# Delta-rule recurrence and two expert layers on one core: joins of the triangular solve in half as many products, the router's weights stored by rows, a longer run of filler products in the routing, and the state's turn ahead of the corner product

## The reference

```python
for t in range(S):
    y[:, :, t] = einsum('bhd,bhde->bhe', r, state)
    Sa = einsum('bhde,bhe->bhd', state, a)
    state = state * w[:, :, None, :] - einsum('bhd,bhe->bhde', Sa, b) + einsum('bhd,bhe->bhde', v, k)
...
e_idx = argmax(x @ w_gate, axis=1)
out[mask] = gate_w[mask, None] * eom[mask, e, None] * (maximum(x[mask] @ w1[e], 0.0) @ w2[e])
...
x = _moe_ref(x=x, **moe_kwargs)
return _moe2_ref(x=x, **moe2_kwargs)
```

## Time and profile before

| | us |
|---|---|
| median of 3 runs | 1289.96 |
| lowest, highest | 1289.43, 1297.5 |
| the profiled execution | 1287.04 |
| its span | 1285.3 |
| PE busy | 1097.9 (85%) |
| VectorE busy | 558.7 (43%) |
| ScalarE busy | 396.4 (31%) |
| GpSimd busy | 302.4 (24%) |

### The profile page before, as it was taken

The page is one execution under the profiler, slowest core; times in us unless marked ns, Lnnn a source line. Parts: engine busy times, 40 slices in busy tenths (PEclk is TensorE's granted clock), DMA queues, the critical chain, the costliest instruction groups (busy, mean ns, idle before and its releaser), DMA issues.

```text
span 1285.3 us, 41335 instructions
## 1 busy us (share of the span) xinstructions
PE 1097.9 (85%) x18328; PEld 949.7 (74%) x18328; DVE 558.7 (43%) x864; ACT 396.4 (31%) x550; POOL 302.4 (24%) x253
## 2 busy tenths in 40 slices
PE   1189894888898889986899999999569999997997
PEld 0188784777888878885788888888448888876885
DVE  6635363364536443416176777767650111110111
ACT  0033332333333334331333333333004333323330
POOL 5440443043034213000112122121201212121111
PEclk8557997896888689777799999999868999998999
DMA  3333439343334333216024224333300331443000
GB/s 84 93 96 84 101 88 68 78 95 81 95 74 110 81 88 74 56 40 199 18 74 146 66 77 129 98 115 103 87 7 29 123 107 61 141 139 112 21 11 1
DMA packets 143115, 107.64 MB, mean 84 GB/s; under 512 B 91553, under 2 KB 120233, under 8 KB 142813
## 3 DMA queue, kind: packets, MB, share of 16 engines
q1 hardware_dynamic: 130560, 84.99, 25.0%
q0 software_dynamic: 6016, 16.05, 3.9%
q10 hardware_dynamic: 6364, 3.96, 2.0%
HBM read 87.51 MB, written 22.09 MB: 85 GB/s over the span
## 4 chain that ended last, share of the span: by engine, by line
PE 76%; DVE 8%; issue 7%; POOL 3%; DMA 3%; ACT 2%; SPq 1%; ACTq 0%; POOLq 0%; DVEq 0%
PE pair L1179 19%; PE pair L1160 17%; PE pair L1167 5%; PE pair L986 4%; PE bank L1054 3%; PE pair L1147 2%; PE pair L875 2%; PE pair L1073 2%; POOL AG L575 2%; PE bank L969 2%; PE bank L1062 2%; PE pair L892 2%; PE pair L924 2%; PE bank L1136 2%; PE pair L909 2%
## 5 line engine op out<-in xcount | busy, mean ns | idle before, releaser
L1179 PE MATMUL pair<-abk_own,H_nat 128*128 x992 | 277.7, 433 | 1.7 <-DVE S_nat L1451 1.7
L1160 PEld LDWEIGHTS pair<-H_nat,rvm 128*128 128x128 f32 x1984 | 238.3, 197 | 23.0 <-ACT H_nat L665 14.2
L1160 PE MATMUL pair<-H_nat,rvm 128*128 128x128 f32 x1984 | 239.6, 281 | 11.9 <-ACT H_nat L665 11.9
L1179 PEld LDWEIGHTS pair<-abk_own,H_nat 128*128 128x128 f32 x992 | 183.9, 190 | 71.3 <-issue 2.7
L665 ACT ACTIVATE rvm<-ring_own 128x2560 f32 x62 | 145.0, 2339 | 149.5 <-issue 86.0
L816 ACT ACTIVATE H_nat<-pair 128x512 f32<-128x512 f32 x62 | 37.0, 596 | 289.4 <-PE pair L1167 289.4
L1451 DVE TENSOR_SCALAR S_nat<-pair,gate_all 128x320 f32<-128x320 f32 x62 | 34.1, 551 | 206.1 <-PE pair L1179 206.1
L1444 DVE TENSOR_SCALAR H_nat<-pair 128x512 f32<-128x512 f32 x62 | 42.5, 686 | 167.0 <-PE pair L1167 167.0
L575 POOL TENSOR_TENSOR AG<-abk_own,F_run 40x512 f32<-40x512 f32 x48 | 60.3, 1257 | 173.9 <-DVE T_nat L1254 143.5
L589 POOL TENSOR_SCALAR_AFFINE_SELECT AG<-AG 64x512 f32<-64x512 f32 x48 | 43.1, 899 | 202.6 <-ACT AG L665 200.2
L646 POOL DMA_INDIRECT between<-S_nat,token_all x31 | 33.9, 1094 | 234.7 <-DVE S_nat L1462 226.6
(11 more groups left out here) (137 smaller groups left out, 1501.2 us busy)
## 6 DMA issues: line engine op xcount, KB each, us to landing
abk_own<-w SPq DMA_DIRECT2D x16, 1280.0 KB, 8.6
ring_own<-w SPq DMA_DIRECT2D x16, 512.0 KB, 3.6
ring_own<-w SPq DMA_DIRECT2D x32, 256.0 KB, 4.6
t_dram<-T_rows SPq DMA_DIRECT2D x12, 384.0 KB, 2.4
ring_own<-w SPq DMA_DIRECT2D x32, 128.0 KB, 5.2
w_in<-wT SPq DMA_DIRECT2D x48, 80.0 KB
abk_own<-aT SPq DMA_DIRECT2D x24, 160.0 KB
abk_own<-bT SPq DMA_DIRECT2D x24, 160.0 KB
```

The lines of the kernel that those rows point to most:

```text
L1160: mm(to, w1_now[:, par, k * F + m * P:k * F + m * P + P], xT[:, (0, 2 - m // 4)[k], :], start=(m % 4 == 0 and k == 0), stop=False, skip_gr ...
L1179: last = mm(bank[5][:, 0:DM], hidT[par][:, k, :], ring2[:, bass.ds(place, 1), k, :].rearrange("p a d -> p (a d)"), start=(k == 0), stop=(k ...
```

## The change

1. **Joins.** `join_first` and `join_second` treat both 32 x 32 blocks of a chunk in one product. Instead of 64 products of 16 x 16 each has 32 of 64 x 32. So that the blocks don't mix, `D_nat` becomes 64 x 64 per head with its two 16 x 16 blocks on the diagonal and zeros elsewhere (cleared once, semaphore `d_cleared`), and GpSimd clears the block of `G_b` with rows 0 to 31 and columns 32 to 63 of each half once per set (`cut_g`, semaphore `g_cut`, for which `join_first` waits). `A_sb` has both blocks' columns, and ScalarE copies 512 instead of 256 columns.
2. **Router.** `load_next_router` stores the weights as they are, 320 rows of 8; `wr_next` is broadcast in that layout, and VectorE's product reads it with a step of 8 numbers.
3. **`WARM`** is 11 instead of 6.
4. **Order.** In `c` = 0 `state_natural` comes ahead of `corner` on PE, and ScalarE's `s_out` ahead of `t10_out`.
5. `lg_parts` keeps two sets' parts instead of all, and ScalarE's copy into it waits for the sum of two sets ago.

```diff
-WARM = 6
+WARM = 11
...
-        D_nat = sb("D_nat", [P, CC * H, BLK])
-        A_sb = sb("A_sb", [P, CC * H, BLK])
+        D_nat = sb("D_nat", [P, CC * H, C])
+        A_sb = sb("A_sb", [P, CC * H, 2, BLK])
...
-        lg_parts = sb("lg_parts", [P, NG, NPAIR, 2 * E])
+        lg_parts = sb("lg_parts", [P, 2, 2, NPAIR, 2 * E])
...
-        wr_dram = nc.dram_tensor("wr_dram", [E, DM], F32, kind="Internal").ap()
+        wr_dram = nc.dram_tensor("wr_dram", [DM, E], F32, kind="Internal").ap()
...
-            sp.dma_start(wr_next, wr_dram.unsqueeze(0).to_broadcast([P, E, DM])).then_inc(wr_landed, 16)
+            sp.dma_start(wr_next, wr_dram.unsqueeze(0).to_broadcast([P, DM, E])).then_inc(wr_landed, 16)
...
+            nc.gpsimd.memset(D_nat[:, :], 0.0).then_inc(d_cleared, 1)
...
+            def cut_g(k):
+
+                pool.wait_ge(gb_copied, k + 1)
+                for h in range(2):
+                    nc.gpsimd.memset(G_b[SIDE[h]:SIDE[h] + HALF, k % 2].rearrange("p c o a t -> p (c o a) t")[:, :, HALF:C],
+                                     0.0).then_inc(g_cut, 1)
+                    pool.wait_ge(g_cut, 2 * k + h + 1)
...
                 if nats:
                     mask_gk(2 * nat_set)
+                if grams:
+                    cut_g(gram_set)
+                if nats:
                     mask_gk(2 * nat_set + 1)
...
-            def turn_router():
-                act.dma_start(wr_dram, router_w[1, :, 0:E].rearrange("d e -> e d"),
-                              allow_slow_non_contiguous=True).then_inc(wr_turned, 16)
+            def load_next_router():
+                act.dma_start(wr_dram, router_w[1, :, 0:E]).then_inc(wr_turned, 16)
...
             def join_first(k):
                 pe.wait_ge(t_landed[k % 2], 16 * T_DMAS * (k // 2 + 1))
+                pe.wait_ge(g_cut, 2 * (k + 1))
...
+                for c in range(CC):
+                    for a in range(NPAIR):
+                        for o in range(2):
+                            for h in range(2):
+                                at = (c * H + o * NPAIR + a) * HALF
+                                q = half_rows(h)
+                                last = mm(pair[1][q, h, at:at + HALF].rearrange("p (m t) -> p m t", m=2),
+                                          G_b[q, k % 2, c, o, a, :],
+                                          T_T[q, (2 * k + c) % 4, o, a, :].rearrange(
+                                              "p (m n t) -> p m n t", m=2, n=2)[:, :, 1, :],
+                                          start=True, stop=True)
...
+                for x in range(CC * H):
+                    for h in range(2):
+                        q = half_rows(h)
+                        last = mm(pair[0][q, h, x * HALF:(x + 1) * HALF], D_nat[q, x, :],
+                                  A_sb[q, x, :, :].rearrange("p m t -> p (m t)"), start=True, stop=True)
...
-                    if c == 0 and chain:
-                        corner(j)
                     if c == 1 and grams:
                         grams_b(j + 2)
                     if chain:
                         state_natural(u)
+                    if c == 0 and chain:
+                        corner(j)
...
-                    v.tensor_tensor(terms, wr_next[:, :, :],
+                    v.tensor_tensor(terms, wr_next.rearrange("p d e -> p e d"),
                                     y_rows[i % 2][:, 0:DM].unsqueeze(1).to_broadcast([P, E, DM]), ALU.mult
```

More of the change, by code:

```diff
@@ L242, in recurrence_and_experts @@
         ring2 = part(abk_own, 0, 2, FC, DM)
-        terms, wr_next = [part(AG[:, :, :, :, :, :].rearrange("p u o b a t -> p (u o b a t)"), n * E * DM, E, DM)
-                          for n in range(2)]
+        A_flat = AG[:, :, :, :, :, :].rearrange("p u o b a t -> p (u o b a t)")
+        terms = part(A_flat, 0, E, DM)
+        wr_next = part(A_flat, E * DM, DM, E)
         w1_now = part(rvm[:, :, :, :, :].rearrange("p n b a t -> p (n b a t)"), 0, 2, W1_COLS)
@@ L463, in fetch_d @@
                     if n % 2 == 0:
-                        sp.dma_start(D_nat[rows_of(h, n), :, :],
+                        sp.dma_start(D_nat[rows_of(h, n), :, n * BLK:(n + 1) * BLK],
                                      tn_dram[k % 2, h, n].rearrange("x t s -> t x s")
@@ L707, in ga_out @@
                 for h in range(2):
-                    copy(A_sb[half_rows(h)].rearrange("p x t -> p (x t)"),
-                         pair[1][half_rows(h), h, 0:CC * H * BLK], ga_copied)
+                    copy(A_sb[half_rows(h)].rearrange("p x m t -> p (x m t)"), pair[1][half_rows(h), h, :], ga_copied)
             def t16_out(k):
@@ L742, in x_out @@
                          pair[2][:, b, :].rearrange("p (a o d) -> p a o d", a=NPAIR, o=2)[:, :, :, 0:D], x_copied)
-                copy(lg_parts[:, 2 * s * NT + t:(2 * s + 1) * NT + t + 1:NT],
+                if k >= 2:
+                    act.wait_ge(lg_summed, k - 1)
+                copy(lg_parts[:, k % 2],
                      pair[2][:, :, :].rearrange("p b (a t) -> p b a t", t=P)[:, :, :, D:D + 2 * E], x_copied)
@@ L796, in _ @@
                     if c == 1 and j == 2:
-                        turn_router()
+                        load_next_router()
             for s in range(2):
@@ L901, in join_first @@
                 pe.wait_ge(gk_copied, 2 * (2 * k + 1))
-                for m in range(2):
-                    for c in range(CC):
-                        for a in range(NPAIR):
-                            for o in range(2):
-                                for h in range(2):
-                                    at = (c * H + o * NPAIR + a) * BLK
-                                    q = SIDE[h] + m * HALF
-                                    last = mm(pair[1][q:q + BLK, h, at:at + BLK],
-                                              G_b[q:q + HALF, k % 2, c, o, a, m * HALF:m * HALF + BLK],
-                                              T_T[q:q + HALF, (2 * k + c) % 4, o, a, m * HALF + BLK:(m + 1) * HALF],
-                                              start=True, stop=True)
+                for c in range(CC):
[9 more added lines that the diff above has]
+                                          start=True, stop=True)
                 last.then_inc(ga_ready, 1)
@@ L919, in join_second @@
                     pe.wait_ge(ut_copied, 2 * k)
-                for m in range(2):
-                    for x in range(CC * H):
-                        for h in range(2):
-                            q = slice(SIDE[h] + m * HALF, SIDE[h] + m * HALF + BLK)
-                            last = mm(pair[0][q, h, x * BLK:(x + 1) * BLK], D_nat[q, x, :], A_sb[q, x, :],
-                                      start=True, stop=True)
+                if k == 0:
+                    pe.wait_ge(d_cleared, 1)
+                for x in range(CC * H):
[3 more added lines that the diff above has]
+                                  A_sb[q, x, :, :].rearrange("p m t -> p (m t)"), start=True, stop=True)
                 last.then_inc(t16_ready, 1)
@@ L1304, in lg_sum @@
                 here = slice(2 * s * NT + t, (2 * s + 1) * NT + t + 1, NT)
-                v.tensor_reduce(lg_all[:, here, :], lg_parts[:, here].rearrange("p g a x -> p g x a"),
+                v.tensor_reduce(lg_all[:, here, :], lg_parts[:, k % 2].rearrange("p g a x -> p g x a"),
                                 AX_X, ALU.add).then_inc(lg_summed, 1)
```

8 lines of the change are left out of this document (6 added, 2 removed).

## The result

| | before | after |
|---|---|---|
| median, us (runs) | 1289.7 (4) | 1331.61 (4) |
| lowest, highest | 1288.81, 1297.5 | 1321.9, 1338.24 |
| ratio, 95% interval | | 1.0305 [1.0229, 1.0382] |
| the profiled execution | 1287.04 | 1329.89 |
| its span | 1285.3 | 1328.1 |

A forecast was written before the change was run, and what follows sets the result against it. TensorE was taken to bound the expert layers; recurrence loops lay 4.7 us above floors of 37.6, from low clock and issue waits. 1287.0 - 18 - 9.2 - 27.5 + 4.0 = 1236.3; forecast 1238 us, range 1211 to 1262.

The forecast's parts named there:

- The price of it: First expert layer: product with wr_next read across takes 4.8 us instead of 2.8, covered except at the end; loss 4.0.
- the 4 us forecast for the end: End of the first expert layer: the last two products, uncovered, each cost 2.0 us more.
- Rival E: First expert layer: reading across also holds back the broadcast operand, product at 9.9 us, kernel slower at 1378; chance 0.02.
- Router, gain 18: Recurrence loop with the router's copy: storing weights as rows removes the long PE wait; gain 18, bounds 16.5 and 21 us.
- Joins, 27.5: Recurrence: 0.8 us of PE time plus 1.7 of waits and clock, 2.5 per loop over 11 loops; bounds 9 and 60.
- Rival A: Recurrence: issue waits have another cause or return elsewhere; joins give 9 instead of 27.5, kernel 1257; chance 0.18.
- 136 packets: Instruction queue: sign of being right, some 136 packets instead of 148, from fewer PE records.
- WARM, 9.2: Both routings: more filler products keep PE's clock up, 48 products take 5.25 us instead of 10.50; gain 4.6 each.
- rival C: Routings: clock stays at 1.2 GHz, 9.2 not gained and 1 to 9 lost, kernel 1248 to 1256; chance 0.07.
- The order, 0: Recurrence: state_natural ahead of corner costs 0, or about 1 us in the first chained slot, as PE has slack there.
- Rivals B: Recurrence: without the burst of joins nearly all waits go and the clock holds, 50 instead of 27.5, kernel 1216; chance 0.17.
- D (1270): First expert layer: product read across costs 6.4 us, VectorE becomes the bound, each tile 1.0 longer, kernel 1270; chance 0.06.

The follow-up runs named there:

- the kernel with the send in time: Changed kernel with the router's weights turned once in SBUF, plus an extra 2.15 us VectorE sum per tile behind the sum releasing the send: 1235.99 us, ratio 0.966.
- the rows-only kernel: Kernel before with only the router's weights stored by rows and read across per tile: 1365.54 us, ratio 1.057.
- the best kernel: Changed kernel with ScalarE turning the router's weights once in SBUF, so the product reads straight: 1238.09 us, ratio 0.957; with the old order 1242.58 us, ratio 0.965.
- the three kernels: Changed kernel with gathers four tiles ahead (1233.44 us), with the router's weights turned once in SBUF (1238.09 us), or with both (1236.45 us).
- the kernel with four pieces: Changed kernel with VectorE's product per tile cut into four of 128 x 640, same reading across: 1262.79 and 1283.31 us.

## Why the prediction was wrong

**The step that failed** is in "The price of it": "8.9 still fit, with 0.6 to spare", and from it "Loss 4.0 (0 to 7.0)". The duration was right, 4.8 us, and so was the sum: VectorE's 8.9 us do fit into 9.5 (in the kernel with the send in time 8.8 us of work cost 2.8 us in the whole layer). What doesn't follow is that nobody waits for them. I asked whether the engine had room and not what hangs on the end of its instruction: the send, and queued behind the send in GpSimd's program the next gather, whose last free place was the 0.6 us ahead of the next product. The loss was 94.5 us instead of 4.0. Of it 57 us are PE's longer waits for rows (61.1 against 4.1), 32 us are PE's records taking longer at clock 0.90 (328.12 - 295.86), and 5 are the rest, in which the 4 us forecast for the end may lie. The layer's price grows with the hold: late with hardly a hold 25 to 45 us, with a hold of 2.3 us 57 (a layer of 366.4), with one of 4.3 us 94.5 (403.5). How the 94.5 divide between the hold and the transfers of weights that a late gather meets stays open.

Rows that would have warned of it were in the trace of before: the gather stands in GpSimd's timeline at 762.13 for 1.02 us, 0.64 us ahead of the product at 763.79. The question to ask of them: move this end by 2.0 us, and what then overlaps what? Even the hold was there once, in the stretch of which the earlier trace rows show a part, where a send meets the product of the last tile:

```profile
920.88 2.82 DVE L1458 TENSOR_TENSOR AG<-AG,S_nat 128x2560 f32<-128x2560 f32 x1
921.15 3.41 POOL L646 DMA_INDIRECT between<-S_nat,token_all  x1 [8.13 <-DVE S_nat L1451]
```

The send takes 3.41 us, where the other 30 of this layer take 1.0 us, and ends 0.86 us after the product.

**Rival E** had the right place and sign but the wrong mechanism. It made VectorE the bound and set the point from which it decides at 7.0 us for the product. The kernel was slower with 4.8.

**Router, gain 18**: right, with 18 us timed (7 to 29) and 19 by the first gather of the rows-only kernel.

**Joins, 27.5**: the size held, 23 us timed (14 to 32), but its two terms were both off. The product's price was outside my bounds: 64 records of the new joins take 1.99 us at clock 1.00, where 126 of the old took 1.62; I had 1.2. From the chain of the changed kernel:

```profile
311.78 1.99 PE pair L926 x64
...
349.87 1.99 PE pair L926 x64
```

So a loop's joins cost about 0.7 us more of PE (twice 1.99 - 1.62), not 0.8 less, and the whole gain is waits and clock. In the nine loops PE's waits for "issue" fall from 30.0 to 11.6 us with the joins alone, and the granted clock rises from 0.82 to 0.91. Waits and clock together then gave about 2.8 us per loop (23 / 11 + 0.7), where I took 1.7. Rival A (the joins give their PE time alone, 9 us) is refuted: that time is negative. A new wait gave some back. In the nine loops of the changed kernel PE waits 14.1 us for GpSimd's scaling, 1.7 before. It comes of joins and order together: it is 1.6 us with the order alone, 5.7 with the joins alone, 1.4 with new joins and the old order in the best kernel, and 7.8 to 19.3 in the kernels that have both. The changed kernel's rows:

```profile
PE pair L873 <- POOL abk_own L588: 14.1, 4, 5.9
PE pair L957 <- ACT T_T L682: 4.9, 8, 0.7
```

The instruction queue brought 136 packets, the number forecast. That the waits are instruction fetch fits all this, but no run here separates fetch from another cost of many small records.

**WARM, 9.2**: the mechanism was right in the trace (one batch of 48 records takes 5.47 us instead of 10.50, the other 5.58), and rival C (the routing's clock stays at 1.2 GHz) is out. The first routing gave 3.7 us from the last sum to the first gather, since the sorting starts 1.3 us later behind the longer row of filler (564.22 - 548.8 = 15.4 us behind that sum, against 607.01 - 592.9 = 14.1); the second 6.2, of which 5.3 come with WARM alone (34.5 - 29.2). That is 9.9 in the pair of traces; timed alone the gain was 2 (from a gain of 7 to a loss of 2), so the term of 9.2 isn't confirmed by time. The batch in the changed kernel, to set beside that of the earlier trace rows:

```profile
564.22 5.47 PE L1155 MATMUL bank<-T_T,F_run 128*128 128x62 f32 x48
```

**The order, 0**: wrong for the kernel before, where it gave 11 us timed; its one trace has a higher clock in the loops. Why, is not settled.

**The sum**: the recurrence got 44.1 us shorter (its last L1092 starts at 545.76, its L1073 at 589.87 before), against 45.5 forecast. With the layer cured, the three kernels run at 0.955 to 0.966 of the kernel before, where 1238 would be 0.960. That is partly luck: timed alone, joins, router, order and WARM gave 23, 18, 11 and 2 us where 27.5, 18, 0 and 9.2 were forecast, and the misses cancel. Rivals B (1216) and D (1270) didn't come.

## What to carry to other kernels

When an instruction gets longer, do not stop at its engine's free time in the beat: follow its end to whoever waits for it, list what is queued behind that waiter on its own engine, and lay those instructions, moved by as much, over the timeline of the other engines. A cover that is counted in busy time says nothing about a transfer that is only issued after it. If such an end must move, fetch one tile further ahead, or put what can wait behind the signal: here the one was worth 98 us (0.0759 of 1290) and the other 56.

## What the runs showed of the hardware

- An indirect gather on GpSimd (DMA_INDIRECT, its indices in SBUF) that starts after VectorE has begun a two-operand TENSOR_TENSOR from SBUF doesn't finish before that: 5.3 us beside the product of 4.8, 3.3 beside the straight one of 2.8, 1.65 beside pieces of 1.25, 1.02 beside none; it ends some 0.9 us after the product or piece. One that starts 0.23 us ahead of the first piece (740.22 in the kernel with four pieces) takes 1.02. A send meets the same: L663 took 5.29 us when it was issued at 965.90, beside the product of 965.62. The Trainium skill (SBUF — State Buffer, section Who interferes with whom) has a port pair shared by VectorE and GpSimd as an exclusive lock, which fits these rows. The same section reports that `tensor_tensor` did not stall DMA in its own test; these rows of an indirect DMA differ, and the measurement decides.
- The record of a gather does not show when its rows are there. They land 1.1 to 2.7 us after its end in the first layer of the kernel before, and 4.2 to 7.1 us after it where the DMA engines are at a share of 0.84 or more (the kernel with four pieces).
- The two engines also lengthen each other in the recurrence, where GpSimd's scaling (L588) takes 2978 ns on average instead of 2413, and VectorE's small copy of `end_decay` (L1247) 1109 instead of 618. In these rows they overlap, and the copy ends as the scaling does. That this is the same lock fits, but no run separates it:

```profile
255.87 2.40 DVE L1242 TENSOR_TENSOR_SCAN E_run<-w_in,ones_at 128x1041 f32<-128x1041 f32 x1
256.17 8.30 POOL L588 TENSOR_TENSOR abk_own<-abk_own,E_run 128x1024 f32<-128x1024 f32 x2
...
258.48 1.78 DVE L1247 COPY end_decay<-E_run 128x16 f32<-128x16 f32 x1
...
260.29 1.99 PE L873 MATMUL pair<-abk_own,AG 64*64 64x64 f32 x64 [5.24 <-POOL abk_own L588]
```

- Reading one operand with 32 bytes between neighbours costs 0.78 ns per element on VectorE on 2560 elements (4820 against 2825 ns), the same as on 192 elements in the kernel before (508 against 358); ScalarE's copy of 2560 read that way takes 4.86 us, a straight one of the experts' weights 2.34.
- Small products don't get cheaper in proportion: in a dense row at clock 1.00, 13 ns per record for 16 x 16 (126 in 1.62 us) and 31 ns for 64 x 32 (64 in 1.99 us), so half as many took longer.
